# Turning the split exponentials by a transposing DMA instead of TensorE and a ScalarE copy, in a fused attention and two-layer expert kernel

## The chip, the core and the metric

The program runs on one core of one Trainium2 chip. The metric is the device time of one execution in microseconds (us); lower is better. The engines are TensorE (PE, with its weight loads shown apart as PEld), VectorE (DVE), ScalarE (ACT), GpSimd (POOL) and SyncE (SP), whose queue issues every DMA of this kernel.

## What is computed

The input x has 2 batches of 11456 points with 128 channels. Stage one is an attention of 32 inducing points over all points of a batch. Stage two is an attention of every point over the 32 results h, then two expert layers in a row, each with 8 experts of width 1024, each point going to its best expert:

```
def mab(q, kv):
    a = exp(s - s.max(-1)), with s = scale * (q @ kv.T)
    return (a / a.sum(-1)) @ kv
h = mab(inducing, x)
attn = mab(x, h)
x1 = gate1 * relu(attn @ w1a[e]) @ w2a[e],  e = argmax of the normalised attn . expert_emb / tau
x2 = gate2 * relu(x1 @ w1b[e]) @ w2b[e],    e = argmax of x1 @ w_gate + bias[modality]
```

## The kernel before, in words

After a setup that reads x twice and forms the weights, the points are worked in 46 chunks of 500 points (4 groups j of 125 points q), 23 for each batch. A step c (from -4 to 45, in a hardware loop for c = 0 to 41) works on five chunks at once, each at another stage: chunk q = c+4 is transposed and scored, chunk p = c+3 gets its attention and its first router, chunk f = c+2 goes through the first expert layer, chunk t = c+1 gets its second router, and chunk c goes through the second layer. Every engine runs its own list of such steps, and semaphores tie them together.

On TensorE a full step has 16 units u: 8 of the second layer (chunk c), then 8 of the first layer (chunk f). A unit is an "up" product into one of four PSUM banks (L1219, three matmuls, for the second layer, L1209, one matmul, for the first), a relu into float16 by ScalarE (L552), the rest of the split by VectorE (L802), and a "down" product of three matmuls (L1196) that waits for it. A step opens with the ups of units 0 to 3, then runs its `start` list, then down(u) and up(u+4) in turn, with small tasks after chosen units: `first_router` after unit 1, `second_router` after 2, `xt` after 4, `scores` after 7, `counts` after 8. TensorE works strictly in this order, so a task that waits holds the rest.

The exponentials of a chunk, `ex`, are split by GpSimd (`gp_step`, L458 and L462) into a high and a low float16 part, each twice, in the tile `E4` (125 points by 4 groups by 128). The attention needs it turned, with the 128 parts on the partitions: `e4`, which is the `start` list, transposes the four groups on TensorE into PSUM (L1231), and ScalarE's task `e4t` copies them to `E4T` (L577, 500 columns, two buffers by the parity of the chunk). `first_router` multiplies `E4T` as weights with the attention values (L1241, L1243), and one step later the ups of the first layer (L1209) read the same buffer as the moving side. Then ScalarE takes squares (L584), GpSimd a power (L485), VectorE the norm (task `norm` after its unit 5, L891 on).

GpSimd goes on after `E4` in `gp_step` with the second router's bias: it waits for the chunk's modality words, makes the bias in five instructions (L468 to L479), and only then comes to the power L485. VectorE's `second_logits` (after its unit 4) waits for that bias at L885.

SyncE's step is `load` of the points of chunk c+4 (L339, 250 KB, once chunk c+3 has been transposed), `loadm` of the modality words of chunk c+1 (L344), and `store` of the result of chunk c-1 (L348), which blocks SyncE until the data is written (L350).

ScalarE opens a step with `yhi` (L572), which waits for the last down of the first layer in the step before; its semaphore is `yhi_ready`.

Of the kernel before, what the change touches and what calls it, by code (L numbers as in the profile page):

```python
# [5 lines left out]
def attention_two_moe_kernel(nc, x, inducing, expert_emb, tau, w1a, w2a, modality_id, w_gate, modality_bias,  # L6
# [25 lines left out]
    NB, NT, C = x.shape  # L32
# [26 lines left out]
    assert NF % UP == 0  # L59
    CW = CT + 4  # L60

    S_W = 2.0 ** 6
# [7 lines left out]
    with ctx:  # L70
# [6 lines left out]
        def sem(name):  # L77
# [9 lines left out]
        ytb = RH[:, BUF0:BUF0 + 4 * CW]  # L87
        E4T = RH[:, BUF0 + 4 * CW:BUF0 + 6 * CW]
        BUF1 = BUF0 + 6 * CW
        hhi, hlo = (RH[:, BUF1 + k * UP * CT:BUF1 + (k + 1) * UP * CT] for k in range(2))  # L90
# [61 lines left out]
        ex = sb("ex", [TQ, TJ, M])  # L152
        E4 = sb("E4", [TQ, TJ, 4, M], f16)
        ss = sb("ss", [TQ, TJ])
# [42 lines left out]
            "chunk_loaded chunk_transposed chunk_xT_ready chunk_scores chunk_max chunk_dif chunk_exp "  # L197
            "e4_hi_ready e4_ready e4_transposed e4t_ready "

# [53 lines left out]
        def run(tasks, slots):  # L253

            for u in slots:
                for task in tasks.get(u, ()):
                    task()

        def parity(c):
            return c % 2 if isinstance(c, int) else c & 1  # L260
# [53 lines left out]
        def _(sp):  # L314
# [31 lines left out]
            def store(z):  # L346
# [4 lines left out]
                sp.sem_inc(s["out_free"], 1)  # L351

            def sp_step(c):
                l2, l1, ry, rx, xq = parts(c)
                if xq:
                    if not isinstance(c, int) or c > -4:
                        sp.wait_ge(s["chunk_transposed"], c + 4)
                    load(c + 4)
                if ry:
                    if not isinstance(c, int) or c > -1:  # L360
                        sp.wait_ge(s["bias_ready"], c + 1)
                    loadm(c + 1)
                if not isinstance(c, int) or c >= 1:
                    store(c - 1)
# [28 lines left out]
        def _(gp):  # L393
# [10 lines left out]
            for m in (ident, ident16):  # L404
# [9 lines left out]
            done(nc.gpsimd.memset(c1[:, :], 0.0))  # L414
            done(nc.gpsimd.memset(xTs[:, :], 0.0))
            done(nc.gpsimd.iota(idx8[:, :], pattern=[[-1, NE]], base=NE, channel_multiplier=0,
                                allow_small_or_imprecise_dtypes=True))
# [29 lines left out]
            gp.wait_ge(s["h_done"], 1)  # L447
            for m in (ytb, E4T):
                nc.gpsimd.memset(m, 0.0).then_inc(s["pads_cleared"], 1)

            def gp_step(c):
                l2, l1, ry, rx, xq = parts(c)
                p, t = c + 3, c + 1
                if rx:
                    gp.wait_ge(s["chunk_exp"], p + 1)
                    if not isinstance(p, int) or p >= 1:
                        hold(gp, "e4_transposed", p)
                    nc.gpsimd.tensor_copy(E4[:, :, 0:2, :],  # L458
                                          ex[:, :, :].unsqueeze(2).to_broadcast([TQ, TJ, 2, M])).then_inc(
                        s["e4_hi_ready"], 1)  # L460
                    gp.wait_ge(s["e4_hi_ready"], p + 1)
                    nc.gpsimd.tensor_tensor(E4[:, :, 2:4, :], ex[:, :, :].unsqueeze(2).to_broadcast([TQ, TJ, 2, M]),  # L462
                                            E4[:, :, 0:2, :], ALU.subtract).then_inc(s["e4_ready"], 1)
                if ry:
                    gp.wait_ge(s["modality_loaded"], 16 * t + 16)
                    hold(gp, "router_steps", CJ * (c + 3))
                    b0 = 5 * t
                    nc.gpsimd.tensor_copy(modf[:, 1, :], modi[:, 0:2 * TJ:2]).then_inc(s["bias_steps"], 1)  # L468
                    hold(gp, "bias_steps", b0 + 1)
                    nc.gpsimd.tensor_scalar(modf[:, 0, :], modf[:, 1, :], -1.0, 1.0, ALU.mult, ALU.add).then_inc(  # L470
                        s["bias_steps"], 1)
                    gp.wait_ge(s["bias_steps"], b0 + 2)
                    for k in range(2):
                        nc.gpsimd.tensor_tensor(bt[:, k, :, :],
                                                biasb[0:TQ, k, :].unsqueeze(1).to_broadcast([TQ, TJ, NE]),
                                                modf[:, k, :].unsqueeze(2).to_broadcast([TQ, TJ, NE]),
                                                ALU.mult).then_inc(s["bias_steps"], 1)
                    gp.wait_ge(s["bias_steps"], b0 + 4)
                    nc.gpsimd.tensor_tensor(bt[:, 2, :, :], bt[:, 0, :, :], bt[:, 1, :, :], ALU.add).then_inc(  # L479
                        s["bias_steps"], 1)  # L480
                    gp.wait_ge(s["bias_steps"], b0 + 5)
                    gp.sem_inc(s["bias_ready"], 1)
                if rx:
                    gp.wait_ge(s["squares_ready"], p + 1)
                    nc.gpsimd.tensor_tensor(st[:, 2, :], ss[:, :], root[0:TQ, :], ALU.pow).then_inc(  # L485
                        s["norm_ready"], 1)
# [5 lines left out]
        def _(act):  # L492
# [33 lines left out]
            for k in range(NB + 4 * NE):  # L526
# [6 lines left out]
                if k >= NB and (k - NB) % 4 == 3:  # L533
# [3 lines left out]
                    nc.scalar.activation(hi, a, ACT.Copy, scale=S_W).then_inc(s["w2b_hi_ready"], 1)  # L537
            act.wait_ge(s["pads_cleared"], 2)

# [26 lines left out]
            def act_step(c):  # L566
# [7 lines left out]

                def e4t():
                    act.wait_ge(s["e4_transposed"], p + 1)
                    nc.scalar.activation(E4T[:, bass.ds(parity(p) * CW, CT)].rearrange("k (j q) -> k j q", q=TQ),  # L577
                                         TB16[:, 0:TJ * (TQ + 1)].rearrange("k (j q) -> k j q", q=TQ + 1)[:, :, 0:TQ],
                                         ACT.Copy).then_inc(s["e4t_ready"], 1)

                def squares():
# [33 lines left out]
                def tasks(after):  # L615
                    return {1: [e4t] if rx else [], 4: [squares] if rx else [], 7: [xt] if xq else [],
                            8: [lexps] if rx or ry else [], 10: [lambda: yt(after())] if l2 else [],
                            13: [exps] if xq else [], 15: [result] if l2 else []}
# [44 lines left out]
        def _(v):  # L663
# [143 lines left out]
            def mask_to(layer, dst, e):  # L807

                n = len(dst)
                for k, d in enumerate(dst):  # L810
                    ins = nc.vector.scalar_tensor_tensor(d, rkb[:, layer, :], idx8[:, bass.ds(e, 1)], xto[:, k, :],
                                                         ALU.is_equal, ALU.mult)
                return ins

            def passes(layer, re, rm, dst, us, tasks):
# [3 lines left out]
                for k, d in enumerate(dst):  # L819
                    ins = nc.vector.tensor_copy(xto[:, k, :], d)  # L820
                ins.then_inc(s["input_kept"], 1)
# [11 lines left out]
            def dve_step(c):  # L833
# [176 lines left out]
                def step(mixed):  # L1010
                    reset()
                    if mixed:
# [9 lines left out]
                        if l1:  # L1022
                            passes(0, re1, rm1, [E4T[:, bass.ds(parity(c) * CW, CT)]], range(NF, 2 * NF), tasks)
                        else:
                            run(tasks, range(NF, 2 * NF))
# [28 lines left out]
        def _(pe):  # L1054
# [131 lines left out]
            def pe_step(c):  # L1186
# [16 lines left out]
                def layer1(woff, opens):  # L1203
                    goff = bounded(pe, half(f) * (NE * F) + (woff >> 1), (NB * NE - 1) * F)
                    woff = bounded(pe, woff, (NE - 1) * 2 * F)
                    eoff = bounded(pe, parity(f) * CW, CW)

                    def up(fb, k):
                        return mm(ups[k][:, 0:CT], G[:, bass.ds(goff + fb * P, P)], E4T[:, bass.ds(eoff, CT)],  # L1209
                                  start=True, stop=True)  # L1210
                    return up, down_of(W2A, woff, y1, opens)
# [14 lines left out]

                def e4():
                    pe.wait_ge(s["e4_ready"], p + 1)
                    for j in range(TJ):
                        o = j * (TQ + 1)  # L1230
                        ins = nc.tensor.transpose(TB16[:, o:o + TQ], E4[:, j, :, :].rearrange("q r m -> q (r m)"),  # L1231
                                                  ident16[0:TQ, 0:TQ])
                    ins.then_inc(s["e4_transposed"], 1)

                def first_router():
                    pe.wait_ge(s["e4t_ready"], p + 1)
                    b = bounded(pe, half(p), NB - 1)
                    eo = bounded(pe, parity(p) * CW, CW)
                    for j in range(TJ):
                        w = E4T[:, bass.ds(eo + j * TQ, P)]  # L1240
                        lg = mm(SM[:, 128 + j * NE:128 + (j + 1) * NE], w, H4f[:, bass.ds(b * (C + NE) + C, NE)],  # L1241
# [52 lines left out]

                start = when(rx, e4)
                tasks = {1: when(rx, first_router), 2: when(ry, second_router), 4: when(xq, xt),
# [79 lines left out]
```

## Time and profile before

| what | value |
|---|---|
| median of 3 runs | 1140.99 us (1136.89 to 1141.04) |
| profiled execution | 1142.4 us, given by its span from the first to the last instruction |
| TensorE busy | 1074.0 us, 94% of the span |
| TensorE, share of the chain that ended last | 91% |
| one full step in the loop | 19.96 to 19.97 us |
| mean granted TensorE clock | 0.973 |

The busy time adds up each engine's instructions. The chain that ended last is followed back from the last instruction, at each point to what released it. The timeline lists instructions in order with the idle time before them in brackets and who ended it. The windows view gives the busy time of each engine in a stretch, the granted clock, and the DMA engines' share.

### The profile page before, as it was taken

To read this page: it belongs to the slowest core of one execution; us is meant where nothing else is said; L and a number is where in the kernel's file an instruction comes from. 1 tells how busy PE (TensorE), PEld (TensorE's weight loads), DVE (VectorE), ACT (ScalarE), POOL (GpSimd) and SP (SyncE) were. 2 spreads that over 40 slices of the span, in tenths; PEclk is the share of its full clock that TensorE was granted. 3 is DMA by queue.
4 is the path that set the end of the run, shared out by engine and by line. 5 is a ranking of instruction groups with operands and counts; after the bars stand their busy time and mean duration, and the time that the engine had idled before them with its cause. 6 is when DMAs were issued, how large, how long until landed. Compare 5 with 4: busy or idle time off the path is not lost.

```text
span 1142.4 us, 29623 instructions
## 1 busy us (share of the span) xinstructions
PE 1074.0 (94%) x6715; PEld 610.7 (53%) x6715; DVE 789.5 (69%) x2342; ACT 724.2 (63%) x1761; POOL 160.9 (14%) x424
## 2 busy tenths in 40 slices
PE   6988876889999999999999999999999999999887
PEld 6987533445555555555555555555555555555443
DVE  4568884557776767777676777767677776767654
ACT  3458663456666666666666766666676666667553
POOL 3100001111111111111111111111111111111100
PEclk9989996889999999999999999999999999999999
DMA  8305650000000000000000000000000000000000
GB/s 332 120 22 163 212 174 21 12 21 27 27 27 27 27 26 20 26 27 27 27 27 27 19 27 27 27 27 27 27 20 26 27 27 27 27 27 18 12 22 20
DMA packets 38288, 52.89 MB, mean 46 GB/s; under 512 B 7504, under 2 KB 24056, under 8 KB 37604
## 3 DMA queue, kind: packets, MB, share of 16 engines
q1 hardware_dynamic: 38244, 52.35, 14.3%
q8 instruction: 22, 0.36, 0.1%
q14 instruction: 22, 0.18, 0.1%
HBM read 40.57 MB, written 11.78 MB: 46 GB/s over the span
## 4 chain that ended last, share of the span: by engine, by line
PE 91%; issue 3%; DVE 2%; ACT 1%; POOL 1%; DMA 1%; ACTq 0%; POOLq 0%; DVEq 0%
PE y L1196 41%; PE up L1219 22%; PE up L1209 7%; PE SM L1273 4%; PE TB L1116 3%; PE y L1092 2%; PE up L1084 2%; PE y L1288 2%; PE TB L1264 2%; PE up L1135 1%; PE TB L1243 1%; PE SM L1255 1%; PE up L1092 1%; PE TB L1231 1%; DMA stage<-in_moe_w 1%
## 5 line engine op out<-in xcount | busy, mean ns | idle before, releaser
L802 DVE SCALAR_TENSOR_TENSOR R<-up,R 128x500 f16<-128x500 f32 x736 | 491.0, 673 | 216.3 <-ACT R L552 216.2
L552 ACT ACTIVATE R<-up 128x500 f16<-128x500 f32 x736 | 416.1, 586 | 146.7 <-PE up L1209 79.1
L1219 PE MATMUL up<-R,W1B 128*128 (+1 forms) x1104 | 277.7, 382 | 21.1 <-issue 15.9
L1196 PE MATMUL y<-R 128*128 128x500 f16 x1104 | 292.1, 373 | 0.4 <-DVE R L802 0.4
L1196 PE MATMUL y<-R,W2A 128*128 128x500 f16 x1104 | 279.5, 375 | 1.3 <-DVE R L802 1.3
L1219 PEld LDWEIGHTS up<-R,W1B 128*128 x1104 | 108.8, 99 | 158.4 <-issue 49.5
L1196 PEld LDWEIGHTS y<-R,W2A 128*128 x1104 | 104.5, 101 | 101.1 <-issue 15.9
L1196 PEld LDWEIGHTS y<-R 128*128 x1104 | 100.3, 97 | 88.3 <-issue 3.1
L1209 PE MATMUL up<-R 128*128 (+1 forms) x368 | 138.3, 379 | 0.0
L485 POOL TENSOR_TENSOR st<-ss,root 125x4 f32<-125x4 f32 x46 | 46.8, 1018 | 386.0 <-ACT TB L584 386.0
L458 POOL CAST E<-ex 125x256 f16<-125x256 f32 x46 | 18.3, 397 | 403.7 <-ACT ex L603 403.7
L611 ACT ACTIVATE SALL<-y,coef 125x128 f32<-125x128 f32 x184 | 52.5, 368 | 33.9 <-PE y L1288 33.9
L584 ACT ACTIVATE TB<-TB 125x128 f32<-125x128 f32 x184 | 48.6, 264 | 28.0 <-PE TB L1243 28.0
L577 ACT ACTIVATE R<-TB 128x500 f16 (+1 forms) x46 | 27.0, 587 | 56.4 <-PE TB L1231 56.4
L1209 PEld LDWEIGHTS up<-R 128*128 x368 | 36.4, 99 | 42.3 <-issue 1.6
L1273 PEld LDWEIGHTS SM<-HT,xTs 128*128 128x128 f32 x368 | 50.8, 202 | 10.4 <-DVEq L909 3.9
L1273 PE MATMUL SM<-HT,xTs 128*128 (+1 forms) x368 | 48.2, 276 | 3.4 <-DVEq L909 2.7
L572 ACT ACTIVATE R<-y 128x500 f32 (+1 forms) x46 | 27.0, 587 | 37.4 <-PE y L1196 37.4
L1116 PE MATMUL TB<-R,pex 128*64 x360 | 44.7, 285 | 5.9 <-ACT pex L511 5.6
L590 ACT ACTIVATE xTs<-TB 128x500 f32<-128x500 f32 x46 | 27.0, 587 | 33.5 <-PE TB L1264 33.5
L501 ACT ACTIVATE W1B<-up 128x512 f32<-128x512 f32 x45 | 26.7, 597 | 34.0 <-PE up L1084 34.0
L1116 PEld LDWEIGHTS TB<-R,pex 128*64 128x64 f32 x360 | 41.7, 144 | 8.9 <-issue 8.8
(149 smaller groups left out, 1136.1 us busy)
## 6 DMA issues: line engine op xcount, KB each, us to landing
stage<-in_moe_w SPq DMA_DIRECT2D x24, 512.0 KB, 3.9
xin<-in_x SPq DMA_DIRECT2D x46, 250.0 KB
out<-SALL SPq DMA_DIRECT2D x46, 250.0 KB
R<-in_x SPq DMA_DIRECT2D x4, 2304.0 KB, 17.5
SALL<-in_moe_w SPq DMA_DIRECT2D x8, 512.0 KB, 4.3
R<-in_x SPq DMA_DIRECT2D x1, 2240.0 KB, 29.6
modi<-in_moe_modality_id SPq DMA_DIRECT2D x46, 3.9 KB
R<-in_x SPq DMA_DIRECT2D x1, 64.0 KB, 29.1
```

What stands on the lines that cost most here:

```text
L485: nc.gpsimd.tensor_tensor(st[:, 2, :], ss[:, :], root[0:TQ, :], ALU.pow).then_inc(s["norm_ready"], 1)
L552: nc.scalar.activation(hhi[:, (u % UP) * CT:(u % UP + 1) * CT], ups[u % UP][:, 0:CT], ACT.Relu).then_inc(s["hi_done"], 1)
L572: nc.scalar.activation(ytb[:, bass.ds(parity(t) * 2 * CW, CT)], y1[:, 0:CT], ACT.Copy, scale=S_Y).then_inc(s["yhi_ready"], 1)
L584: ins = nc.scalar.activation(TB[0:TQ, j * C:(j + 1) * C], TB[0:TQ, j * C:(j + 1) * C], ACT.Square, accum_out=ss[:, j:j + 1])
L611: ins = nc.scalar.activation(yout[:, j * C:(j + 1) * C], y2[0:TQ, j * C:(j + 1) * C], ACT.Copy, scale=coef[:, bass.ds(parity(c) * TJ + j, 1)])
L802: nc.vector.scalar_tensor_tensor(hlo[:, o:o + CT], ups[u % UP][:, 0:CT], 0.0, hhi[:, o:o + CT], ALU.max, ALU.subtract).then_inc(s["lo_done ...
L1092: ins = mm(sbank(k)[:, j * M:(j + 1) * M], xsT[:, k, j * P:(j + 1) * P], indT[:, :], start=True, stop=True)
L1116: ins = mm(hp, pex[:, k, j, :], R[:, bass.ds((g * GT + j) * C, C)], start=False, stop=False, skip_group_check=True)
L1196: ins = mm(y[:, 0:CT], W[:, bass.ds(woff + (fb * 2 * C + o), C)], h[:, k * CT:(k + 1) * CT], start=opens and fb == 0 and n == 0, stop=fb = ...
L1209: return mm(ups[k][:, 0:CT], G[:, bass.ds(goff + fb * P, P)], E4T[:, bass.ds(eoff, CT)], start=True, stop=True)
L1219: ins = mm(ups[k][:, 0:CT], W1B[:, bass.ds(woff + (wl * F + fb * P), P)], ytb[:, bass.ds(yoff + yl * CW, CT)], start=n == 0, stop=n == 2)
L1273: ins = mm(SM[:, j * M:(j + 1) * M], xTs[:, j * TQ:j * TQ + P], HT[:, bass.ds(bounded(pe, half(q) * M, (NB - 1) * M), M)], start=True, sto ...
```

## The change

`E4` gets 128 partitions, cleared once in GpSimd's setup, so that its last three rows stay zero. A new function `turn` on SyncE, first in `sp_step`, issues one transposing DMA from `E4` to `E4T`. It waits for `e4_ready` of the chunk, and, from chunk 2 on, for `yhi_ready` p-1, which tells that the first layer has finished with the buffer. TensorE's `e4` and ScalarE's `e4t` are gone; `first_router` waits for the DMA's count. `E4T` now holds 128 columns for each group, of which 125 are points, so its readers get an access of 4 runs of 125 (`points`). The other hunks of the diff rename sizes and give VectorE's branch for mixed experts the same access.

```
+            def turn(p):
+                hold(sp, "e4_ready", p + 1)
+                if not isinstance(p, int) or p >= 2:
+                    hold(sp, "yhi_ready", p - 1)
+                sp.dma_start_transpose(E4T[:, bass.ds(parity(p) * EW, EW)].rearrange("k (j q) -> k j q", q=P),
+                                       E4[:, :, :, :].rearrange("q j r m -> q (j r m)")).then_inc(s["e4t_ready"], 16)
+
             def sp_step(c):
                 l2, l1, ry, rx, xq = parts(c)
+                if rx:
+                    turn(c + 3)
                 if xq:
                     if not isinstance(c, int) or c > -4:
                         sp.wait_ge(s["chunk_transposed"], c + 4)
                     load(c + 4)
...
+            done(nc.gpsimd.memset(E4[:, :, :, :], 0.0))
...
-            for m in (ytb, E4T):
-                nc.gpsimd.memset(m, 0.0).then_inc(s["pads_cleared"], 1)
+            nc.gpsimd.memset(ytb, 0.0).then_inc(s["pads_cleared"], 1)
...
-                        hold(gp, "e4_transposed", p)
+                        hold(gp, "e4t_ready", 16 * p)
...
-                def e4t():
-                    act.wait_ge(s["e4_transposed"], p + 1)
-                    nc.scalar.activation(E4T[:, bass.ds(parity(p) * CW, CT)].rearrange("k (j q) -> k j q", q=TQ),
-                                         TB16[:, 0:TJ * (TQ + 1)].rearrange("k (j q) -> k j q", q=TQ + 1)[:, :, 0:TQ],
-                                         ACT.Copy).then_inc(s["e4t_ready"], 1)
...
-                        return mm(ups[k][:, 0:CT], G[:, bass.ds(goff + fb * P, P)], E4T[:, bass.ds(eoff, CT)],
-                                  start=True, stop=True)
+                        return mm(ups[k][:, 0:CT].rearrange("p (j q) -> p j q", q=TQ), G[:, bass.ds(goff + fb * P, P)],
+                                  points(E4T[:, bass.ds(eoff, EW)]), start=True, stop=True)
...
-                def e4():
-                    pe.wait_ge(s["e4_ready"], p + 1)
+                def first_router():
+                    pe.wait_ge(s["e4t_ready"], 16 * p + 16)
+                    b = bounded(pe, half(p), NB - 1)
+                    eo = bounded(pe, parity(p) * EW, EW)
                     for j in range(TJ):
-                        o = j * (TQ + 1)
-                        ins = nc.tensor.transpose(TB16[:, o:o + TQ], E4[:, j, :, :].rearrange("q r m -> q (r m)"),
-                                                  ident16[0:TQ, 0:TQ])
-                    ins.then_inc(s["e4_transposed"], 1)
...
-                start = when(rx, e4)
+                start = []
```

## Rows read from the trace of the kernel before

**Rows 1.** The page: busy time by engine, and the last chain by engine.

```profile
PE 1074.0 (94%) x6715; PEld 610.7 (53%) x6715; DVE 789.5 (69%) x2342; ACT 724.2 (63%) x1761; POOL 160.9 (14%) x424
...
PE 91%; issue 3%; DVE 2%; ACT 1%; POOL 1%; DMA 1%; ACTq 0%; POOLq 0%; DVEq 0%
```

**Rows 2.** Windows of one step each: length, busy by engine, granted clock, DMA share, GB/s.

```profile
642.70:662.66 19.96, 19.83 (x127) 10.55 (x126) 14.50 (x44) 13.55 (x35) 3.09 (x9) 1.00 0.09 26
```

**Rows 3.** Timeline of a step, TensorE: start, duration, engine, line, operation, tiles, count.

```profile
645.19 2.69 PE L1219 MATMUL up<-R,W1B 128*128 x12
...
647.72 0.39 PE L1231 MATMUL TB<-ident,E 125*128 125x125 f16 x4
...
647.94 0.80 PE L1196 MATMUL y<-R 128*128 128x500 f16 x3
...
650.26 0.10 PEld L1241 LDWEIGHTS SM<-H,R 128*128 x1
...
654.47 0.59 PE L1264 MATMUL TB<-ident,xin 125*128 125x125 f32 x4
...
656.59 0.80 PE L1196 MATMUL y<-R 128*128 128x500 f16 x3
```

**Rows 4.** Timeline of the same step, ScalarE.

```profile
645.34 0.59 ACT L572 ACTIVATE R<-y 128x500 f32 x1 [0.75 <-PE y L1196]
...
648.38 0.59 ACT L577 ACTIVATE R<-TB 128x500 f16 x1 [1.14 <-PE TB L1231]
```

**Rows 5.** Timeline of the same step, DMA issues on SyncE's queue.

```profile
655.44 0.27 SPq L339 DMA_DIRECT2D xin<-in_x  x1
...
656.16 0.26 SPq L344 DMA_DIRECT2D modi<-in_moe_modality_id  x1
```

**Rows 6.** Timeline of the same step, GpSimd.

```profile
652.28 1.02 POOL L485 TENSOR_TENSOR st<-ss,root 125x4 f32<-125x4 f32 x1 [8.30 <-ACT TB L584]
...
661.91 0.67 POOL L462 TENSOR_TENSOR E<-ex,E 125x256 f16<-125x256 f32 x1
...
662.53 0.19 POOL L468 CAST modf<-modi 125x4 f32<-125x4 int32 x1
...
663.70 0.25 POOL L479 TENSOR_TENSOR bt<-bt 125x32 f32<-125x32 f32 x1
```

**Rows 7.** Timeline of the same step, VectorE.

```profile
652.89 0.19 DVE L885 TENSOR_TENSOR LG<-u,bt 125x32 f32<-125x32 f32 x1
...
653.60 0.15 DVE L891 SCALAR_TENSOR_TENSOR st<-st 125x4 f32<-125x4 f32 x1
...
655.47 0.67 DVE L802 SCALAR_TENSOR_TENSOR R<-up,R 128x500 f16<-128x500 f32 x1
```

**Rows 8.** Windows after the two issues of rows 5, columns as in rows 2.

```profile
656.80:659.20 2.40, 2.40 (x17) 1.51 (x16) 1.99 (x5) 1.64 (x3) 0.00 (x0) 1.00 0.29 99
659.20:659.60 0.40, 0.40 (x7) 0.25 (x7) 0.40 (x4) 0.32 (x1) 0.00 (x0) 1.00 0.20 28
659.60:660.00 0.40, 0.40 (x4) 0.17 (x2) 0.40 (x2) 0.27 (x1) 0.00 (x0) 1.00 0.03 1
```

**Rows 9.** DMA view, 80 to 90 us: GB/s in 40 slices; issues with us to landing.

```profile
GB/s 12 78 78 47 119 299 344 352 342 297 129 0 0 0 0 0 0 0 0 0 63 156 106 80 260 340 348 342 295 103 4 0 31 90 143 125 244 352 342 352
...
stage<-in_moe_w SPq DMA_DIRECT2D x2, 512.0 KB, 3.9
```

**Rows 10.** Timelines of steps -3 and -1: GpSimd and TensorE, then ScalarE and TensorE.

```profile
169.10 0.67 POOL L462 TENSOR_TENSOR E<-ex,E 125x256 f16<-125x256 f32 x1
...
171.11 0.19 PE L1241 MATMUL SM<-H,R 128*128 128x8 f16 x1 [0.68 <-ACT R L577]
...
196.47 0.59 ACT L572 ACTIVATE R<-y 128x500 f16<-128x500 f32 x1 [2.44 <-PE y L1196]
...
198.81 0.18 PE L1241 MATMUL SM<-H,R 128*128 128x8 f16 x1 [0.68 <-ACT R L577]
```

**Rows 11.** Timeline of TensorE where the loop has ended: a step's first ups.

```profile
1067.61 4.35 PE L1219 MATMUL up<-R,W1B 128*128 128x500 f16 x12 [3.25 <-issue]
```

More of the change, by code:

```diff
@@ L60, in attention_two_moe_kernel @@
     CW = CT + 4
+    EW = TJ * P
     S_W = 2.0 ** 6
@@ L87, in attention_two_moe_kernel @@
         ytb = RH[:, BUF0:BUF0 + 4 * CW]
-        E4T = RH[:, BUF0 + 4 * CW:BUF0 + 6 * CW]
-        BUF1 = BUF0 + 6 * CW
+        E4T = RH[:, BUF0 + 4 * CW:BUF0 + 4 * CW + 2 * EW]
+        BUF1 = BUF0 + 4 * CW + 2 * EW
         hhi, hlo = (RH[:, BUF1 + k * UP * CT:BUF1 + (k + 1) * UP * CT] for k in range(2))
@@ L152, in attention_two_moe_kernel @@
         ex = sb("ex", [TQ, TJ, M])
-        E4 = sb("E4", [TQ, TJ, 4, M], f16)
+        E4 = sb("E4", [P, TJ, 4, M], f16)
         ss = sb("ss", [TQ, TJ])
@@ L197, in attention_two_moe_kernel @@
             "chunk_loaded chunk_transposed chunk_xT_ready chunk_scores chunk_max chunk_dif chunk_exp "
-            "e4_hi_ready e4_ready e4_transposed e4t_ready "
+            "e4_hi_ready e4_ready e4t_ready "
             "att_done squares_ready norm_ready yhi_ready ylo_ready modality_loaded bias_steps bias_ready "
@@ L257, in run, with points @@
                     task()
+        def points(a):
+            return a.rearrange("k (j q) -> k j q", q=P)[:, :, 0:TQ]
         def parity(c):
@@ L456, in gp_step @@
                     if not isinstance(p, int) or p >= 1:
-                        hold(gp, "e4_transposed", p)
-                    nc.gpsimd.tensor_copy(E4[:, :, 0:2, :],
+                        hold(gp, "e4t_ready", 16 * p)
+                    nc.gpsimd.tensor_copy(E4[0:TQ, :, 0:2, :],
                                           ex[:, :, :].unsqueeze(2).to_broadcast([TQ, TJ, 2, M])).then_inc(
@@ L461, in gp_step @@
                     gp.wait_ge(s["e4_hi_ready"], p + 1)
-                    nc.gpsimd.tensor_tensor(E4[:, :, 2:4, :], ex[:, :, :].unsqueeze(2).to_broadcast([TQ, TJ, 2, M]),
-                                            E4[:, :, 0:2, :], ALU.subtract).then_inc(s["e4_ready"], 1)
+                    nc.gpsimd.tensor_tensor(E4[0:TQ, :, 2:4, :], ex[:, :, :].unsqueeze(2).to_broadcast([TQ, TJ, 2, M]),
+                                            E4[0:TQ, :, 0:2, :], ALU.subtract).then_inc(s["e4_ready"], 1)
                 if ry:
@@ L537, in _ @@
                     nc.scalar.activation(hi, a, ACT.Copy, scale=S_W).then_inc(s["w2b_hi_ready"], 1)
-            act.wait_ge(s["pads_cleared"], 2)
+            act.wait_ge(s["pads_cleared"], 1)
             npas = act.alloc_register("act_pass")
@@ L615, in tasks @@
                 def tasks(after):
-                    return {1: [e4t] if rx else [], 4: [squares] if rx else [], 7: [xt] if xq else [],
+                    return {4: [squares] if rx else [], 7: [xt] if xq else [],
                             8: [lexps] if rx or ry else [], 10: [lambda: yt(after())] if l2 else [],
@@ L810, in mask_to @@
                 for k, d in enumerate(dst):
-                    ins = nc.vector.scalar_tensor_tensor(d, rkb[:, layer, :], idx8[:, bass.ds(e, 1)], xto[:, k, :],
-                                                         ALU.is_equal, ALU.mult)
+                    r, x0 = rkb[:, layer, :], xto[:, k, :]
+                    if layer == 0:
+                        r, x0 = (a.rearrange("p (j q) -> p j q", q=TQ) for a in (r, x0))
+                    ins = nc.vector.scalar_tensor_tensor(d, r, idx8[:, bass.ds(e, 1)], x0, ALU.is_equal, ALU.mult)
                 return ins
@@ L819, in passes @@
                 for k, d in enumerate(dst):
-                    ins = nc.vector.tensor_copy(xto[:, k, :], d)
+                    x0 = xto[:, k, :]
+                    ins = nc.vector.tensor_copy(x0.rearrange("p (j q) -> p j q", q=TQ) if layer == 0 else x0, d)
                 ins.then_inc(s["input_kept"], 1)
@@ L1022, in step @@
                         if l1:
-                            passes(0, re1, rm1, [E4T[:, bass.ds(parity(c) * CW, CT)]], range(NF, 2 * NF), tasks)
+                            passes(0, re1, rm1, [points(E4T[:, bass.ds(parity(c) * EW, EW)])], range(NF, 2 * NF), tasks)
                         else:
@@ L1205, in layer1 @@
                     woff = bounded(pe, woff, (NE - 1) * 2 * F)
[L1206 removed]
+                    eoff = bounded(pe, parity(f) * EW, EW)
                     def up(fb, k):
[L1209 to L1210 removed]
+                        return mm(ups[k][:, 0:CT].rearrange("p (j q) -> p j q", q=TQ), G[:, bass.ds(goff + fb * P, P)],
+                                  points(E4T[:, bass.ds(eoff, EW)]), start=True, stop=True)
                     return up, down_of(W2A, woff, y1, opens)
@@ L1225, in layer2 @@
                     return up, down_of(W2B, woff, y2, opens, before if opens else None)
-                def e4():
-                    pe.wait_ge(s["e4_ready"], p + 1)
+                def first_router():
+                    pe.wait_ge(s["e4t_ready"], 16 * p + 16)
+                    b = bounded(pe, half(p), NB - 1)
+                    eo = bounded(pe, parity(p) * EW, EW)
                     for j in range(TJ):
-                        o = j * (TQ + 1)
-                        ins = nc.tensor.transpose(TB16[:, o:o + TQ], E4[:, j, :, :].rearrange("q r m -> q (r m)"),
-                                                  ident16[0:TQ, 0:TQ])
-                    ins.then_inc(s["e4_transposed"], 1)
[L1235 to L1240, printed above, removed]
+                        w = E4T[:, bass.ds(eo + j * P, P)]
                         lg = mm(SM[:, 128 + j * NE:128 + (j + 1) * NE], w, H4f[:, bass.ds(b * (C + NE) + C, NE)],
```

## The prediction, on record before the changed kernel ran

> **What bounds the kernel now.** I read the page first: TensorE is busy 94% of the span and holds 91% of the chain that ended last [rows 1]. Windows of one step each show whether that is even: 41 of them in a row are alike, 19.96 us with 19.83 us of TensorE at full granted clock [rows 2]. So in the loop a microsecond that TensorE waits is one on the time, and only its own instructions removed give anything back. The timeline of one step then gives the places. I count times from that step's first up (645.19, called 0): transposes L1231 at 2.53, the next down at 2.75, `first_router` at 5.07, down of unit 7 at 11.40 [rows 3].
>
> **What is removed.** The four transposes take 0.22 us from their first start to the down behind them [rows 3]; the 0.39 us of the row counts a modelled end. That is in 43 steps with work around it (c = 0 to 42) 9.5 us. ScalarE's copy of 0.59 us [rows 4] goes too; TensorE did not wait for it there, since it ended at 3.78, 1.3 us ahead of `first_router`, so I give it nothing. Removing all else than the transposes cannot speed up a TensorE that is busy 19.83 of 19.96 us. The cleared `E4` and the reads in runs of 125 I take as free: the clearing lies in the setup, beside the loading of x, and the matmul reads the same 500 columns. A matmul of this access is in no row; if its 8 ups a step cost a tenth of a 0.21 us column stream more, that is 7 us in all, and I keep it inside the range.
>
> **When the transfer can start.** `E4` is ready before the step begins: L462 ends at 662.58, that is 2.6 us before the next step [rows 6]. But `turn` also waits for `yhi_ready`, which L572 gives at 0.74 [rows 4]. From the end of what SyncE waits for to its DMA there are 0.38 us (L1264 ends at 655.06, the load starts at 655.44) [rows 3, 5]. So the transfer starts at 1.12. `first_router` wants it at 5.07 - 0.22 = 4.85. The allowance is 3.73 us from issue to landing.
>
> **What the transfer takes.** No row shows a transposing DMA, nor one from on-chip memory. From below: a load of 512 KB lands 3.9 us after its issue, and the rate in the middle is about 350 GB/s [rows 9], so 1.5 us are data and 2.4 us fixed; 128 KB at that rate are 0.37 us, together 2.8 us. From above: these weights come in packets of 512 bytes, 23 ns each on one of 16 DMA engines at that rate (350/16 = 21.9 GB/s). If the turned side is written in 32-byte pieces and none is cheaper than such a packet, 256 pieces an engine take 6.0 us, together 8.4 us. Neither end is nearer in kind, so I take the geometric middle of the data times 0.37 and 6.0, which is 1.5 us, and with 2.4 fixed 3.9 us to landing. Less than the plain load I exclude, since nothing in turning makes it faster.
>
> At 3.9 us the data come at 5.02, only 0.17 us after `first_router` wants them. So the direct wait is small. It isn't the whole price.
>
> **What is queued behind `turn`.** Before, SyncE issued the loads of step c+1 in the middle of step c, at 10.25 and 10.97 [rows 5], because only `xt` held them. Now they stand behind `turn` in SyncE's program and can't go before 1.12 of the next step. With the spacing of 0.72 us between two DMAs with their address work [rows 5], `load` goes at 1.84, `loadm` at 2.56. The points keep time: they land some 4 us later, at about 5.9, and `xt` wants them near 9. The modality words don't. The data of the pair run from 656.8, and the small tail with the last packets lies in 659.2 to 660.0 [rows 8], so the modality words land 3.4 to 3.8 us after their issue, behind the points on the same queue. So they land at 5.96 to 6.36, middle 6.16, in place of long before the step.
>
> Who waits for that: GpSimd's bias is 1.42 us long (662.53 to 663.95), and the power L485 of 1.02 us stands behind it [rows 6]. VectorE's norm L891 waits for the power, and from L891's start at 8.41 to the end of the L802 of unit 7 at 10.95 it works without a gap, 2.54 us [rows 7]. Down of unit 7 wants that at 11.40 - 0.22 = 11.18. So L891 must start by 8.64, the power end by 8.60, the bias end by about 7.5 (0.1 us for semaphores), and the modality words land by 5.95. The slack is gone already with the plain load: 6.16 is 0.2 us late. L885 wants the bias at 7.70 - 0.22, the same bound.
>
> With 1.5 us of turning data in front, the points' data, which would begin about 0.7 us after those of the turn, are pushed by 0.8 us: the modality words land at 6.94, 1.0 us late. The same comes out if SyncE, instead of the DMA engines, is what the turn keeps busy. The wait of 0.17 at `first_router` lies within this 1.0, since it moves TensorE and so the deadline. Per step 1.0 - 0.22 = +0.78 us, times 43 = +34 us.
>
> **The steps ahead of the loop.** In steps -3 to -1 nothing covers the transfer. Before, from the end of L462 to `first_router` were 1.34 us (169.77 to 171.11), and from the end of L572 1.75 us in step -1 [rows 10]. Now they are 0.38 + 3.9 = 4.28: +2.9 twice and +2.5, together +8 us. In step 0 TensorE's entry into the loop covers it.
>
> **Sum.** -9.5 + 43 + 8 = +42 us (43 being 43 times 1.0). The profiled execution has 1142.4 us, 1.4 above the median; I add to the median: 1141 + 42 = 1183 us.
>
> By the Trainium skill (Advanced Engine Details and Errata, X-Bar Transpose (TRN2)) transposing DMAs here are as fast as regular ones, which stands by the lower end of 2.8 us; no row before the change can show it. By it the time would be that of rival A. The Trainium skill (VectorE: DVE Perf Modes, The three transpose paths) gives a 128x128 of two bytes 1309 ns by the DMA crossbar and 390 ns by TensorE, and so speaks against the change. Four blocks in a row would be an estimated 5.2 us of data; it would lead to rival B. The trace agrees in so far as TensorE's four here cost 0.22 us of the stream.
>
> **Rivals.**
>
> A. *The transfer is as cheap as a plain load, and the change is not slower.* 2.8 us fits in the allowance of 3.73. What decides is whether the modality words land before or after 5.95. At 5.96 to 6.36 each step gets 0.0 to 0.4 us of wait, net -0.2 to +0.2, times 43 = -9 to +9 us; the early steps cost +5 (1.84 + 1.6 + 1.44). That is 1137 to 1155 us. With the on-chip source a little quicker than memory it is the lower part, and down to 1134 if the early steps cost nothing. For it speaks the idle DMA: its share is 0.09 of a step [rows 2]. Against it: 2.4 us fixed and the order of SyncE's queue hold whatever the data rate.
>
> B. *The turning is long, in small pieces or block by block.* TensorE then waits in `first_router` itself. At 6.0 us to landing the wait there is 2.27 us, the modality words are late by 0.83 more (the points follow the turn's data), net 2.9 a step, +124 and +15 early: 1280 us. At 8.4 us it is 4.67 + 0.83 - 0.22 = 5.3 a step, +227 and +22: 1390 us. There the idle of 4.7 us is longer than the 3.25 us before L1219 at 1067.61, whose twelve matmuls took 4.35 us in place of 2.69 [rows 3, 11]; such a half clock behind every wait would add up to 1.66 times 43 = 71 us, to 1461. For it speaks that 128 rows must be gathered for every row written; against it, nothing in the trace.
>
> C. *The DMA doesn't turn in large pieces at all but writes each 2-byte element.* 4096 elements an engine at 23 ns are 96 us in every step, beyond anything that hides: about 5000 us.
>
> **Chances and range.** Forecast (3.2 to 5 us to landing, 1150 to 1225 us): 0.48, of which 0.02 within 0.5%. A: 0.23, of which 0.10 faster by over 0.5% and 0.13 within (what of it ends above 1146.7 us is counted with the forecast). B: 0.26. C: 0.03. A measurement of this kernel can tell about 0.5%, that is 5.7 us, from no change: below 1135.3 is faster, above 1146.7 slower. So faster 0.10, same 0.15, slower 0.75. The range must take in A's middle and B up to some 7 us to landing (1280 + 1.0 times 43 + 3 = 1326): 1136 to 1335 us. The forecast's own part is 1150 to 1225.
>
> **What the profile after would show.** L1231 and L577 gone, each step shorter by 0.22 us where nothing waits. SyncE's transposing DMA at 1.1 us into the step and its load 0.7 us or more behind it; if the gap is much longer, the turn costs issue time. TensorE idle before L1241, released by a DMA, of about 0.2 us (much more: B; none: A). GpSimd's L468 no longer right behind L462 but released by the modality load at 6 to 7 us into the step, then L885 or L891 on VectorE waiting for GpSimd, and TensorE's downs near unit 7 waiting for VectorE, 1 us a step. Wrong would be the forecast if GpSimd's bias still lies ahead of the step, or if L891 waits and no down does, or if the wait at L1241 is over 1 us.

## The result and the profile after

The changed kernel takes 1208.03 us, the median of 4 runs (1206.85 to 1208.75); the kernel before, run beside it, 1138.94 us (1136.51 to 1141.04). The ratio is 1.058, with a 95% interval from 1.055 to 1.062: slower by 69 us. The prediction was slower by 42 us, 1183 us, with a range that holds the result. The profiled execution of after has a span of 1205.1 us and a time of 1206.85 us. The span of the profiled one of before, 1142.4 us, lies above all four of its times, so the two profiles differ by 62.7 us only. The split further down is made within those 62.7.

The page of after: busy time, the last chain by engine, and the new DMA with its time to landing.

```profile
PE 1080.0 (90%) x6531; PEld 601.8 (50%) x6531; DVE 789.9 (66%) x2342; ACT 711.1 (59%) x1715; POOL 162.9 (14%) x424
...
PE 57%; DMA 10%; issue 9%; DVE 7%; POOL 7%; SPq 5%; ACT 3%; POOLq 1%; DVEq 0%; ACTq 0%
...
R<-E SPq DMA_TRANSPOSE x46, 2.4
```

Against [rows 1] TensorE's share of the last chain fell from 91% to 57%, and DMA (10% against 1%), GpSimd (7% against 1%) and SyncE's queue (5%) have grown in it, a sign of a new wait in every step.

One step of after in the timeline, TensorE. It begins at 656.17, the next at 677.34: 21.17 us, one of the shortest (they vary from 21.17 to 21.91).

```profile
656.17 2.69 PE L1230 MATMUL up<-R,W1B 128*128 x12
...
658.70 0.80 PE L1207 MATMUL y<-R 128*128 128x500 f16 x3
...
661.02 0.10 PEld L1244 LDWEIGHTS SM<-H,R 128*128 x1
...
661.23 0.17 PE L1244 MATMUL SM<-H,R 128*128 x1
...
666.06 0.80 PE L1207 MATMUL y<-R 128*128 128x500 f16 x3 [0.24 <-DVE R L810]
...
667.46 0.80 PE L1207 MATMUL y<-R 128*128 128x500 f16 x3 [0.39 <-DVE R L810]
...
668.77 0.80 PE L1207 MATMUL y<-R 128*128 128x500 f16 x3 [0.29 <-DVE R L810]
...
677.34 2.69 PE L1230 MATMUL up<-R,W1B 128*128 x12
```

Counted from the step's start, the first down comes at 2.53 where it came at 2.75 [rows 3]: the 0.22 us of the transposes are saved. `first_router` loads its first weights at 4.85, as forecast, and its first matmul starts at 5.06, with no wait for the DMA. The three downs of units 5, 6 and 7 wait for VectorE. Down of unit 7 comes at 12.60; before it was 11.40, and 11.18 is what the saving would make it. So this step loses 1.42 us there. The three brackets add up to 0.92 us and tell only part of it, since the profile models the ends of matmuls.

SyncE, GpSimd and VectorE in the same step:

```profile
657.26 1.22 SPq L362 DMA_TRANSPOSE R<-E  x1
...
659.02 0.29 SPq L344 DMA_DIRECT2D xin<-in_x  x1
659.82 0.27 SPq L349 DMA_DIRECT2D modi<-in_moe_modality_id  x1
...
663.42 0.19 POOL L482 CAST modf<-modi 125x4 f32<-125x4 int32 x1 [9.82 <-DMA modi<-in_moe_modality_id]
...
664.60 0.25 POOL L493 TENSOR_TENSOR bt<-bt 125x32 f32<-125x32 f32 x1
665.03 1.02 POOL L499 TENSOR_TENSOR st<-ss,root 125x4 f32<-125x4 f32 x1 [0.18 <-POOL bt L493]
...
665.13 0.19 DVE L896 TENSOR_TENSOR LG<-u,bt 125x32 f32<-125x32 f32 x1 [1.52 <-POOLq L496]
...
666.08 0.16 DVE L902 SCALAR_TENSOR_TENSOR st<-st 125x4 f32<-125x4 f32 x1 [0.16 <-POOL st L499]
...
667.96 0.67 DVE L810 SCALAR_TENSOR_TENSOR R<-up,R 128x500 f16<-128x500 f32 x1
```

The transposing DMA starts at 1.09, as forecast (1.12). It keeps SyncE for 1.22 us, where an ordinary DMA takes 0.27 [rows 5]. So the load of the points follows 1.76 us after the turn's start, not 0.72, and the modality words go at 3.65. They reach GpSimd at 7.25. From there the chain is the one of the prediction: bias, power (L499), norm (L902 at 9.91, deadline 8.64), unit 7 (ends at 12.46), down of unit 7. Against [rows 6] GpSimd's L482 no longer stands behind the split of `E4` but 9.82 us after it.

The data of the transposing DMA in windows (length, busy by engine, clock, DMA share, GB/s):

```profile
658.40:658.80 0.40, 0.40 (x4) 0.19 (x2) 0.40 (x2) 0.40 (x1) 0.00 (x0) 1.00 0.78 159
658.80:659.20 0.40, 0.40 (x4) 0.18 (x2) 0.40 (x2) 0.35 (x2) 0.00 (x0) 1.00 0.83 168
...
658.60:659.00 0.40, 0.40 (x4) 0.24 (x3) 0.40 (x2) 0.35 (x2) 0.00 (x0) 1.00 1.10 219
```

All but a small tail is through by 659.2, 1.9 us after the start of the issue and before the first of the points' data. The last window, which lies across the other two, shows all DMA engines busy and 219 GB/s. The waits of the whole execution, in sum, times and the longest, say that this is every step's story and that the turned data themselves are waited for only three times, in the early steps:

```profile
DVE LG L896 <- POOLq L496: 79.2, 42, 4.1
...
PE y L1207 <- DVE R L810: 52.4, 130, 1.0
...
PEld SM L1244 <- DMA R<-E: 14.8, 3, 6.2
```

Where the 62.7 us went, by the starts of the first ups of steps: from step 2 to step 41 before 265.82 to 1044.52, after 269.14 to 1107.43, so 39 steps of 19.97 us became 39 of 21.49, +59.6 us; ahead of step 2 +3.3; behind step 41 -0.2.

### The profile page after: what moved, and what is told of

Same layout as the page of the kernel before. It is cut to its first block, busy times and chain, and to the rows that moved or that the text cites. A ratio compares the mean times of both kernels' runs of the same rounds, so it can differ in the third digit from the quotient of the medians.

```text
span 1205.1 us, 29341 instructions
## 1 busy us (share of the span) xinstructions
PE 1080.0 (90%) x6531; PEld 601.8 (50%) x6531; DVE 789.9 (66%) x2342; ACT 711.1 (59%) x1715; POOL 162.9 (14%) x424
## 4 chain that ended last, share of the span: by engine, by line
PE 57%; DMA 10%; issue 9%; DVE 7%; POOL 7%; SPq 5%; ACT 3%; POOLq 1%; DVEq 0%; ACTq 0%
PE y L1207 27%; PE up L1230 9%; DMA modi<-in_moe_modality_id 8%; PE up L1220 4%; PE SM L1276 3%; SPq L362 3%; PE TB L1127 3%; DVE R L810 3%; POOL st L499 3%; PE y L1103 2%; PE up L1095 2%; PE y L1291 2%; DMA stage<-in_moe_w 1%; ACT R L586 1%; POOL bt L488 1%
## 5 line engine op out<-in xcount | busy, mean ns | idle before, releaser
L1230 PE MATMUL up<-R,W1B 128*128 (+1 forms) x1104 | 273.5, 377 | 16.6 <-issue 11.6
L1207 PEld LDWEIGHTS y<-R 128*128 x1104 | 104.1, 97 | 166.3 <-issue 106.1
L619 ACT ACTIVATE SALL<-y,coef 125x128 f32<-125x128 f32 x184 | 52.5, 368 | 33.9 <-PE y L1291 33.9
L482 POOL CAST modf<-modi 125x4 f32<-125x4 int32 x46 | 8.6, 186 | 464.4 <-DVE u L890 303.7
L896 DVE TENSOR_TENSOR LG<-u,bt 125x32 f32<-125x32 f32 x46 | 8.9, 193 | 79.3 <-POOLq L496 79.2
L499 POOL TENSOR_TENSOR st<-ss,root 125x4 f32<-125x4 f32 x46 | 46.8, 1018 | 27.5 <-ACT TB L592 20.0
L602 ACT ACTIVATE lex<-ld 125x64 f32<-125x64 f32 x48 | 12.3, 256 | 60.6 <-DVE ld L923 60.5
```

The lines of the kernel that those rows point to most:

```text
L619: ins = nc.scalar.activation(yout[:, j * C:(j + 1) * C], y2[0:TQ, j * C:(j + 1) * C], ACT.Copy, scale=coef[:, bass.ds(parity(c) * TJ + j, 1)])
L1207: ins = mm(y[:, 0:CT], W[:, bass.ds(woff + (fb * 2 * C + o), C)], h[:, k * CT:(k + 1) * CT], start=opens and fb == 0 and n == 0, stop=fb = ...
L1230: ins = mm(ups[k][:, 0:CT], W1B[:, bass.ds(woff + (wl * F + fb * P), P)], ytb[:, bass.ds(yoff + yl * CW, CT)], start=n == 0, stop=n == 2)
```

## Experiments

All are compared with the kernel before on the same chip. "Words" are the modality words, the "turn" is the transposing DMA, and a spare turn is one whose result nobody reads. For each I give the ratio, and the length of a step as the first ups of steps 2 and 41, divided by 39.

**The two loads ahead of the turn.**

```
-                if rx:
-                    turn(c + 3)
                 if xq:
                     if not isinstance(c, int) or c > -4:
                         sp.wait_ge(s["chunk_transposed"], c + 4)
                     load(c + 4)
                 if ry:
                     if not isinstance(c, int) or c > -1:
                         sp.wait_ge(s["bias_ready"], c + 1)
                     loadm(c + 1)
+                if rx:
+                    turn(c + 3)
```

> The changed kernel with load and loadm ahead of turn in SyncE's step, as they stood before. Theory (queue order): the points and the modality words are again issued in the middle of the step before, GpSimd's bias lies ahead of the step, and VectorE's L896 and L902 no longer wait; each step is the 19.97 us of before less the 0.22 us of the transposes, 19.75 us; the time about 1133 us, 0.5% under before. Rival 1 (the transposing transfer or the reads in runs of 125 disturb TensorE or the memory): steps stay near 21.5 us, about 1208 us. Rival 2 (the turned data come too late for first_router once nothing else is late): TensorE waits at L1244 for the DMA in every step.

Measured: 1134.27 us, ratio 0.994 (0.991 to 0.996). The steps, by the first ups of steps 2 and 41:

```profile
266.39 2.69 PE L1230 MATMUL up<-R,W1B 128*128 x12
...
1036.67 2.69 PE L1230 MATMUL up<-R,W1B 128*128 x12
```

That is 19.75 us a step. The 0.22 us come out in full, `first_router` does not wait in the loop, and the strided reads of `E4T` cost nothing that shows. So the loss in the loop hangs on the order on SyncE's queue; both rivals fall.

**Only the modality words ahead of the turn.** `loadm` first, then `turn`, then `load`.

```
+                if ry:
+                    if not isinstance(c, int) or c > -1:
+                        sp.wait_ge(s["bias_ready"], c + 1)
+                    loadm(c + 1)
                 if rx:
                     turn(c + 3)
...
                     load(c + 4)
-                if ry:
-                    if not isinstance(c, int) or c > -1:
-                        sp.wait_ge(s["bias_ready"], c + 1)
-                    loadm(c + 1)
```

> The changed kernel with loadm ahead of turn, and load still behind it. Theory (it is the modality words alone): bias early, steps of about 19.75 us, the time as with both loads ahead, about 1133 to 1136 us; the points land at about 7 us into the step, before xt wants them at 8.9. Rival (the late points set the pace): steps stay above 21 us and TensorE waits at L1267 for the load.

Measured: 1133.3 us, ratio 0.993 (0.991 to 0.996), 19.75 us a step. The points, now issued at 2.9 us into the step, are in time. It is the modality words alone.

**Only the points ahead of the turn.** `load` first, then `turn`, then `loadm`.

```
-                if rx:
-                    turn(c + 3)
                 if xq:
...
                     load(c + 4)
+                if rx:
+                    turn(c + 3)
                 if ry:
```

> The changed kernel with load ahead of turn and loadm behind it. The modality words are issued at about 2.9 us into the step, with no points in front of them in the queue. Theory, with the second half of the price being the 250 KB in front: they land some 2.4 us later, at 5.3, before the 5.9 that the chain allows, so steps of 19.75 to 19.9 us and about 1134 to 1141 us. If the place behind turn alone costs the time, they land at 6.3 or later and steps are 20.1 us or more, 1150 us or more.

Measured: 1135.03 us, ratio 0.994 (0.992 to 0.996), 19.75 us a step. Here the words are issued behind the turn, and yet they are in time:

```profile
704.95 0.27 SPq L349 DMA_DIRECT2D modi<-in_moe_modality_id  x1
...
706.79 0.19 POOL L482 CAST modf<-modi 125x4 f32<-125x4 int32 x1 [7.34 <-DVE st L877]
```

With no points just in front in the queue they reach GpSimd 1.84 us after their issue; in the step of after it was 3.60 behind the points. (The profile puts this wait down to a VectorE instruction long done; the DMA is what came last.) So the loss takes three things together: the wait in `turn`, the turn's time on SyncE, and 250 KB of points in front of 4 KB that are urgent.

**The wait without the DMA.** The kernel before, with `turn`'s two waits at the head of SyncE's step.

```
+                if rx:
+                    hold(sp, "e4_ready", c + 4)
+                    if not isinstance(c, int) or c >= -1:
+                        hold(sp, "yhi_ready", c + 2)
```

> The kernel before (TensorE's transposes and ScalarE's copy in place), with turn's two waits, e4_ready and yhi_ready, at the head of SyncE's step, and no transposing DMA. Theory: the points go at 1.4 us and the modality words at 2.1 us into the step and land at 5.5, within the allowance of 6.2, so the wait alone costs 0 to 0.2 us a step and the time is 1139 to 1148 us; the 1.2 us that SyncE is busy with the transposing DMA is needed for the loss. Rival (the wait alone is what costs, the DMA is innocent): steps near 21.5 us, about 1205 us.

Measured: 1154.55 us, ratio 1.010 (1.007 to 1.014), beyond the 1139 to 1148 expected. A step has 20.06 us, +0.09; that is 4 us in the loop, and step 2 begins 8.1 us later than before (273.95 against 265.82). The words land later than I took:

```profile
716.15 0.26 SPq L344 DMA_DIRECT2D modi<-in_moe_modality_id  x1
...
719.99 0.19 POOL L472 CAST modf<-modi 125x4 f32<-125x4 int32 x1 [8.38 <-DMA modi<-in_moe_modality_id]
```

That is 3.84 us in this step, and the start of the bias varies between 5.67 and 6.53 us into the step, about the deadline, so some steps wait and most don't (13 and 23 of the 36 looked at).

**The wait and a transposing DMA that nobody needs.** As the last one, and behind the waits a DMA of 128x512 from a weight tile to a spare tile. This adds work and takes none away; TensorE still makes the transposes.

```
+                    sp.dma_start_transpose(spare[:, :].rearrange("k (j q) -> k j q", q=P),
+                                           W2A[:, 0:TJ * P]).then_inc(s["spare_turned"], 16)
```

> The kernel before, its own transposes kept, with turn's two waits at the head of SyncE's step and behind them a transposing DMA of the same size from a weight tile to a spare tile that nobody reads. Theory: SyncE's 1.2 us with it (and 0.5 us of address work behind it) put the modality words at 7.0 us into the step as in the changed kernel, and the chain behind them sets the step whatever TensorE does, so steps of about 21.5 us and about 1205 us in all. Rival (part of the loss comes from the turned data's own way, E4T and first_router): steps stay near the 20.06 us of the kernel with the wait alone.

Measured: 1225.37 us, ratio 1.071 (1.067 to 1.074), 21.72 us a step. The mechanism holds: a transposing DMA with no reader costs 1.66 us a step more than the wait alone. The total is 20 us above the 1205 expected. In the loop 9 us of it are the 0.23 us a step above after, in the bias starting later (7.79 against 7.55 us, next table), though the words are issued a little earlier; why they take longer these runs do not show. Step 2 begins at 274.88, 5.7 us later than in after.

**Four buffers for `E4T`.** After's own order; `turn` need not wait for the first layer.

```
-                if not isinstance(p, int) or p >= 2:
-                    hold(sp, "yhi_ready", p - 1)
+                if not isinstance(p, int) or p >= 4:
+                    hold(sp, "yhi_ready", p - 3)
...
-                sp.dma_start_transpose(E4T[:, bass.ds(parity(p) * EW, EW)].rearrange("k (j q) -> k j q", q=P),
+                sp.dma_start_transpose(E4T[:, bass.ds(quarter(p) * EW, EW)].rearrange("k (j q) -> k j q", q=P),
```

> The changed kernel in its own order on SyncE, with four buffers for E4T in place of two, so that turn waits for yhi_ready of two steps earlier, long given, and goes as soon as E4 is ready, 2.2 us before the step. Theory: the modality words go at about 0.3 us and land at 4.1 to 4.8, before 5.9, so steps of 19.75 us, about 1136 us in all. Rival (the 1.2 us on SyncE's queue are the loss wherever they lie): steps of 21 us.

Measured: 1135.97 us, ratio 0.992 (0.990 to 0.995), 19.75 us a step. The turn costs SyncE the same 1.24 us, but it starts 2.1 us ahead of the step; the loss is gone without any change of order. The words still stand behind turn and points here and reach GpSimd 3.9 us after their issue, as in after, but all of it is early. So the 1.2 us hurt only where they stand in front of something due.

The mean start of the bias (GpSimd's first instruction on the words) in the steps between 280 and 1020 us, counted from the step's first up, against the step:

| kernel | words issued | bias starts | step | step less bias start |
|---|---|---|---|---|
| after | 3.65 | 7.55 | 21.49 | 13.94 |
| wait alone | 1.97 | 6.00 | 20.06 | 14.06 |
| wait and spare turn | 3.53 | 7.79 | 21.72 | 13.93 |
| points first | 2.94 | 4.70 | 19.75 | not bound by it |
| four buffers | 0.49 | 4.43 | 19.75 | not bound by it |

Where the bias starts late, the step ends about 13.94 us after it, whoever makes the transposes, and this holds step by step: in after the start varies from 7.26 to 7.97 us, and the end of the step keeps its distance of 13.90 to 13.96. That puts the deadline at 19.97 - 13.94 = 6.03 us where TensorE makes the transposes, and at 19.75 - 13.94 = 5.81 where they are gone. The kernel with the wait alone shows the first of the two directly: its 23 steps with a bias start up to 6.01 take 19.97 us, its 13 steps with a later start (6.05 to 6.53) take longer and end 13.93 to 13.97 us after it.

**Two spare turns ahead of the real one,** both loads ahead of all three.

```
+                for k in range(2):
+                    sp.dma_start_transpose(spare[:, k, :].rearrange("k (j q) -> k j q", q=P),
+                                           W2A[:, 0:TJ * P]).then_inc(s["spare_turned"], 16)
                 sp.dma_start_transpose(E4T[:, bass.ds(parity(p) * EW, EW)].rearrange("k (j q) -> k j q", q=P),
```

> Both loads ahead of turn, and two further transposing DMAs of the same size to spare tiles issued right before the real one, behind the same waits. The real one is issued 2.5 us later, at 3.6 us into the step. Theory: transfers take 2.5 us from issue to release and their issues add up, so the data come at 6.1 to 6.2 us, 1.3 us after first_router wants them (4.85); TensorE waits at L1244 for the DMA, one for one: steps of 21.05 us, about 1195 us in all. The bias plays no part. Rival (two more transfers cost more than their issue, or contend with TensorE's reads): steps well over 21.3 us. Rival 2 (issue times overlap with landing): steps under 20.5 us.

Measured: 1228.02 us, ratio 1.072 (1.069 to 1.076), 21.82 us a step, so 2.07 above 19.75 where 1.3 was expected. One step, from 1060.96 on:

```profile
1061.82 2.52 SPq L364 DMA_TRANSPOSE R<-W2A  x2
1064.57 1.19 SPq L366 DMA_TRANSPOSE R<-E  x1
...
1067.42 0.18 PE L1251 MATMUL SM<-H,R 128*128 x1 [1.24 <-DMA R<-E]
...
1068.14 0.80 PE L1214 MATMUL y<-R 128*128 128x500 f16 x3
```

The real turn starts at 3.61 as worked out, and TensorE's first matmul behind it comes 2.85 us after that, at 6.46 in place of 5.06: 1.40 us of wait. So the direct wait exists, and comes with these 2.5 us of added delay. The rest is behind it: from the first of `first_router`'s matmuls to the next down 0.72 us, where the step of after has 0.32 (661.23 to 661.55), and from the first matmul of `second_router` (L1265, twelve of them) to the next down 0.58, where after has 0.30 (L1258). Why the small matmuls run wider apart after such a wait, these runs do not settle. The granted clock is 1.00 in all windows of it, and not every wait for a DMA does it: in step -1 of after, ahead of the loop, TensorE waits 3.15 us at the same place, and the eight matmuls behind take 0.34 us.

**Transposing DMAs of other sizes.** Both loads ahead, and behind each store three more, 128x128, 128x256 and 128x1024.

```
+                    for k, n in enumerate((1, 2, 8)):
+                        sp.dma_start_transpose(spare[:, k, 0:n * P].rearrange("k (j q) -> k j q", q=P),
+                                               W2A[:, 0:n * P]).then_inc(s["spare_turned"], 16)
```

> Both loads ahead of turn, and in each step three further transposing DMAs behind the store, 128x128, 128x256 and 128x1024 from a weight tile to spare tiles, to see how SyncE's time with one grows with its size; the one of 128x512 takes 1.22 us. Theory (SyncE spends its time block by block): about 0.5, 0.7 and 2.2 us, on a line with 1.22. Rival (a fixed price for any transposing DMA): all near 1.2 us. They lie where SyncE has nothing due, so steps stay at 19.75 to 19.8 us in either case, about 1136 us in all; if the transfers as such disturb TensorE, steps are longer.

Measured: 1133.67 us, ratio 0.991 (0.988 to 0.994), 19.75 us a step. The first, the second, and the last two together on SyncE's queue, from three narrow windows:

```profile
707.52 1.13 SPq L384 DMA_TRANSPOSE R<-W2A  x1
```

```profile
708.70 1.23 SPq L384 DMA_TRANSPOSE R<-W2A  x1
```

```profile
708.70 2.58 SPq L384 DMA_TRANSPOSE R<-W2A  x2
```

So 1.13, 1.23 and, with a gap of 0.05 taken off, 1.30 us for eight times the data of the first; over all steps the means are 1.15, 1.26 and 1.31. My theory of a price by block fell; SyncE's time for one is all but fixed. With three more transposing DMAs a step, 3.7 us of SyncE's time, and no loss, the transfers as such do not disturb TensorE where they lie here.

**Modality words ahead and four buffers.** Both edits at once; the core of them:

```
+                if ry:
+                    if not isinstance(c, int) or c > -1:
+                        sp.wait_ge(s["bias_ready"], c + 1)
+                    loadm(c + 1)
                 if rx:
                     turn(c + 3)
...
-                if not isinstance(p, int) or p >= 2:
-                    hold(sp, "yhi_ready", p - 1)
+                if not isinstance(p, int) or p >= 4:
+                    hold(sp, "yhi_ready", p - 3)
```

> The changed kernel with loadm ahead of turn, load behind it, and four buffers for E4T. In the loop nothing waits in either of the two edits alone, so together steps stay at 19.75 us; only the early steps can gain, where turn no longer waits for yhi_ready: about 1131 us, within 0.3% of the kernel with loadm ahead alone (1133 us).

Measured: 1134.21 us, ratio 0.991 (0.989 to 0.993), 19.75 us a step. The interval overlaps those of the two edits alone; the early steps gain nothing that the times can tell, though in the profiled executions step 2 begins 2.5 us earlier than with the words ahead alone (263.49 against 265.98). All six kernels in which the words come in time and no spare turn stands ahead of the real one have steps of 19.75 us and are 0.6 to 0.9% under the kernel before, each with an interval below 1.

## Why the prediction was right, and which terms were off

The direction and the mechanism held, step by step: TensorE bound; 0.22 us a step saved; `turn` held until 1.1 us by `yhi_ready`; `first_router` not waiting; the modality words late behind `turn` and the points; then bias, power, norm and the down of unit 7. What was off are sizes, and in two places a right size came by another way than forecast. In the profiled executions the loop from step 2 on cost 59.6 us over 39 steps and what lies ahead 3.3, where the sum had 0.78 us for each of 43 steps and 8 ahead:

- *The transfer, "3.9 us to landing".* It lands in 2.4 us by the profile's page, below my lower end of 2.8. The estimate by the plain load from memory was too high even as a floor, and "less than the plain load I exclude" was wrong. So the wait of 0.17 us at `first_router` did not come, and rival B never was near. By the Trainium skill (Advanced Engine Details and Errata, X-Bar Transpose (TRN2)) transposing DMAs are as fast as regular ones, and 350 to 400 GB/s are to be expected. The trace agrees in the time to landing, which is not above the 2.8 us estimated for a plain load, and disagrees in the rate: with all DMA engines busy the window above shows 219 GB/s, less than the 350 of the plain load in [rows 9].
- *"The spacing of 0.72 us between two DMAs with their address work".* This is the step that failed in size. I gave the transposing DMA the issue time of an ordinary one and put all its price on the DMA engines (+0.8 us). SyncE is busy 1.22 us with it and the spacing is 1.76 us: +1.04. The push on the DMA engines did not happen: the turn's data were through before those of the points began. I had noted that it comes to the same if SyncE is what is kept busy, and it does, but for the size. That 0.8 lies near 1.04 is luck, since it was worked out from a transfer taken too long.
- *The words' way, "3.4 to 3.8 us after their issue".* Measured 3.9 on average in after, up to GpSimd's start (3.65 to 7.55). The deadline for the start of the bias is 5.8 where mine was 6.05 (landing at 5.95 and 0.1 for the semaphore). Together: late by 7.55 - 5.8 = 1.75 us in place of 1.0. Less the 0.22 that is 1.53, against my 0.78 and a measured 21.49 - 19.97 = 1.52. The agreement is no check where the 5.8 is taken from the late steps themselves; the check is the kernel with the wait alone, whose steps begin to wait between 6.01 and 6.05, that is 5.8 with the 0.22 taken off.
- *The early steps, +8 us.* The first ups of step 0 do begin 8.8 us later (225.93 against 217.15), but luck is in it. The sum put all 8 on `first_router` waiting for a transfer of 3.9 us. In the traces the transfer is shorter, and in steps -3 and -1 TensorE waits for the load of the points behind the turn too, which the sum left out:

```profile
175.30 1.09 PE L1267 MATMUL TB<-ident,xin 125*128 125x125 f32 x4 [2.21 <-DMA xin<-in_x]
...
207.30 1.10 PE L1267 MATMUL TB<-ident,xin 125*128 125x125 f32 x4 [2.34 <-DMA xin<-in_x]
```

From the first `xt` of step -4 to step 0 the kernel before takes 52.5 us, after 60.9, and the kernel with the two loads ahead of the turn 57.3. So by this comparison some 4.8 us are the turn's and 3.6 come from the loads standing behind it. By step 2 only 3.3 us are left: with the later start, entering the loop cost TensorE less (no 4.71 us gap ahead of step 1, and no half clock behind it). Why the gap is less was not tried.

Rival A, the change not slower, fell by its own point: the words reach GpSimd at 7.55 on average, long after 5.95. But its size for the transfer was nearer (2.8 against 2.4 measured), and with another order of the three DMAs the change is not slower, as the experiments show. The Trainium skill's 1309 ns for a 128x128 (VectorE: DVE Perf Modes, The three transpose paths) would have led, four blocks in a row, to an estimated 5.2 us of data; here 128x512 is through 1.9 us after the start of its issue, and the sizes run shows that SyncE's time does not add up by blocks.

## What to carry to other kernels

When a DMA is put ahead of others on a queue, list everything behind it, with its deadline. Here the smallest transfer, with the earliest reader, mattered, and not the largest: 4 KB of modality words set the length of some 40 steps. A DMA that must wait for this step's work belongs behind the prefetches of the next, or needs more buffers so that it need not wait; in this kernel either turned a loss of 6% into a gain of 0.6 to 0.9%. The turn was not tried on another engine's queue.

## What the runs showed of the hardware that was not expected

A transposing DMA occupies SyncE's queue for 1.13 us at 128x128, 1.23 at 128x256, 1.22 at 128x512 and 1.30 at 128x1024, against 0.26 to 0.29 us for an ordinary DMA. From the start of its issue to landing it takes 2.4 us (128x512, on-chip to on-chip). With all DMA engines busy its data go at 219 GB/s. A DMA of 4 KB reaches its reader 1.8 us after issue with no load just in front, and 3.9 us behind 250 KB of the same queue. After a DMA wait of 1.2 us inside the loop TensorE's next eight small matmuls and the twelve behind took about 0.7 us longer than without it, at full granted clock; after one of 3.15 us ahead of the loop the eight did not. The cause is open.
